# A third buffer for the split expert tiles, and end keys kept in the buffer of the inverse decays

## The chip, the core and the metric

The kernel runs on one core of a Trainium2 chip. The metric is device time in microseconds (us), the median of repeated runs. One more execution was recorded by the hardware profiler; all rows below come from it, and the times in them count from the start of its span. Engines: PE is the matrix engine (TensorE), PEld its weight loads, DVE is VectorE, ACT is ScalarE, POOL is GpSimd, SP issues DMAs.

## The reference

Three layers, one after the other. First a linear attention with decay over 4 batches, 8 heads, 768 tokens and a head width of 48:

```
for t in range(S):
    cur = einsum('bhd,bhe->bhde', u * k[t], v[t])
    y[t] = einsum('bhd,bhde->bhe', r[t], state + cur)
    state = w[t][..., None] * state + einsum('bhd,bhe->bhde', k[t], v[t])
```

Its output, 3072 tokens by 384, goes through a first expert, and that one's output through a second:

```
h = x @ w_in;  e = exp(h - max(h));  solu = h * e / (sum(e) + 1e-9)      # 384 -> 1024
x = ((solu - mean) / sqrt(var + 1e-6) * g_ln) @ w_out                    # 1024 -> 384
h = x @ w_in2; out = maximum(0.01 * h, h) @ w_out2                       # 384 -> 2048 -> 384
```

## The kernel before

**Tiles and stages.** The attention is worked in 24 chunks of 128 tokens (6 per batch), m counting them. Three chunks form a super tile of 384 tokens, which is what the experts' matmuls stream. One super tile takes 24 steps on PE: 8 steps of the kind M1 (the second matmul of the first expert) and 16 of the kind M2 (the second expert). f is the step within its kind, fp numbers all steps of a batch.

**A step.** `prod` writes a tile of 128 features by 384 tokens into one of two PSUM banks, PR[fp % 2]: in M2 nine matmuls of X2 by w_in2 (a product in high and low parts, so three matmuls for each of three blocks), in M1 three transposes of LN. ACT and DVE then split the tile into a high part RH and a low part RL:

- M2, four operations in a chain: ACT writes 0.01 times the tile to Rraw (L693), DVE takes the maximum with the tile (L967), ACT rounds that to RH (L697), DVE writes the rest to RL (L974). Rraw and RL are the same memory.
- M1, two operations: ACT writes gain times the tile to RH (L699), DVE writes the rest to RL (L976).

`cons` multiplies RH and RL by w_out (nine matmuls, summed in the banks ACC) and counts up the semaphore pe_cons. PE's order is prod(fp), cons(fp-2), prod(fp+1), cons(fp-1), and so on; at the end of the M1 steps, and after the last step of all, the pending cons are done in a row. RH, RL and Rraw have two buffers, fp % 2, so ACT's first operation on a tile has two waits (L690 and L691):

```
wait(act, pe_prod, steps(b, fp))
wait(act, pe_cons, steps(b, fp - 2))
```

**The attention beside the steps.** The work of a chunk is cut into 8 slots, which lists written in the program hang between the steps, several per step in the first 16 M2 steps (the opening). For chunk m the slots have: the masked scores A on DVE (L848, slot 4), the product with A on PE (slot 5), the sum y on DVE (L861, slot 6), its transposes on PE (L1155, slot 7), the split of x (ACT L649 and DVE XL L885, slot 7), and the first matmul of the first expert, `expert_in`, 18 matmuls of 512 columns (slot 8). Behind it PE transposes the end keys of the next chunk (L1162). The maximum of the rows (L892, L895), the exponentials on ACT (L625) and their product with h on DVE (L902) follow in slot 8; in an M2 step ACT issues its L693 before that L625.

**Decays, inverse decays, end keys.** For the next chunk DVE writes the running product of the decays (`decay`, L827), its inverse ki (`inverse`, L835, four instructions), and keys times ki into the keys (`undecayed_keys`, L840). After that ACT reads ki and the decays once each to sum them up, with `junk` as the unused output (`take_range`, L656), and POOL writes keys times the last decay into a tile of its own, ke (`end_keys`, L506), which PE transposes.

**The opening.** Weights are split into high and low parts while the first steps run. ACT writes the high parts (L621) and DVE the low parts (`low_part`, L985, two operands read from SBUF, 768 columns at a time), of which the last are written in the first 16 M2 steps.

Each engine has one queue, worked in order, and all waits are semaphores written by hand.

Of the kernel before, what the change touches and what calls it, by code (L numbers as in the profile page):

```python
# [96 lines left out]
def build(nc, rkw, r_tok, k_tok, v_tok, u, w_in1, w_out1, g_ln, w_in2, w_out2,  # L97
          r_ch, k_ch, w_ch, v_ch, u_ch, y_pair, out):
    with ExitStack() as ctx:
# [36 lines left out]
        RH = sb("RH", [128, 2, ST], F32R)  # L136
        RL = sb("RL", [128, 2, ST], F32R)
        Rraw = sb("Rraw", [128, 2, ST], F32, over="RL")
# [11 lines left out]
        ke = sb("ke", [PD, PAIRS, CH])  # L150
        ki = sb("ki", [PD, PAIRS, CH])
        junk = sb("junk", [PD, PAIRS, CH])
# [61 lines left out]
        def decays(b, m):  # L214
            return part(2, b, m)

# [278 lines left out]
        def _(pool):  # L495
# [6 lines left out]
            def end_keys(b, m):  # L502
                wait(pool, dve_keys, chunks(b, m, PAIRS, PAIRS))
                wait(pool, pe_keT, chunks(b, m))
                last = decays(b, m)[:, :, CH - 1:CH].broadcast_to([PD, PAIRS, CH])
                nc.gpsimd.tensor_tensor(ke[:, :, :], keys(b, m), last, ALU.mult).then_inc(pool_ke, 1)  # L506
# [108 lines left out]
        def _(act):  # L615
# [35 lines left out]
            def take_range(b, m):  # L651

                wait(act, dve_inv, chunks(b, m, PAIRS, PAIRS))
                for i, part in enumerate((ki[:, :, :], decays(b, m))):
                    wait(act, act_range, chunks(b, m, 2, i))
                    nc.scalar.activation(junk[:, :, :], part, ACT.Copy,  # L656
                                         accum_out=spread[:, bass.ds(chunks(b, m, 2, i), 1)]).then_inc(act_range, 1)
# [29 lines left out]
            def step(b, kind, so, f, fp, m, s):  # L687
                if kind == "M1":
                    item_mid(b, m, s)
                wait(act, pe_prod, steps(b, fp))  # L690
                wait(act, pe_cons, steps(b, fp - 2))  # L691
                if kind == "M2":
                    nc.scalar.activation(Rraw[:, fp % 2, :], PR[fp % 2][:, 0:ST], ACT.Copy,  # L693
                                         scale=0.01).then_inc(act_slope, 1)
                    item_mid(b, m, s)
                    wait(act, dve_relu, supers(b, so, F2, f + 1))
                    nc.scalar.activation(RH[:, fp % 2, :], Rraw[:, fp % 2, :], ACT.Copy).then_inc(act_hi, 1)  # L697
                else:
                    nc.scalar.activation(RH[:, fp % 2, :], PR[fp % 2][:, 0:ST], ACT.Identity,  # L699
                                         scale=gain[:, f:f + 1]).then_inc(act_hi, 1)  # L700
# [118 lines left out]
        def _(dve):  # L819
# [11 lines left out]
            def inverse(b, m, a):  # L831
                if a == 0:
                    wait(dve, act_range, chunks(b, m, 2))
                wait(dve, dve_decay, chunks(b, m, PAIRS, a + 1))
                nc.vector.reciprocal(ki[:, a, :], decays(b, m)[:, a, :]).then_inc(dve_inv, 1)  # L835
# [129 lines left out]
            def step_relu(b, so, f, fp):  # L965
                wait(dve, act_slope, supers(b, so, F2, f + 1))
                nc.vector.tensor_tensor(Rraw[:, fp % 2, :], PR[fp % 2][:, 0:ST], Rraw[:, fp % 2, :],  # L967
                                        ALU.max).then_inc(dve_relu, 1)

            def step_lo(b, kind, f, fp):  # L970
                wait(dve, act_hi, marks(b, fp))
                hi = RH[:, fp % 2, :].bitcast(F32)
                if kind == "M2":
                    nc.vector.tensor_tensor(RL[:, fp % 2, :], Rraw[:, fp % 2, :], hi, ALU.subtract).then_inc(dve_lo, 1)  # L974
                else:
                    nc.vector.scalar_tensor_tensor(RL[:, fp % 2, :], PR[fp % 2][:, 0:ST], gain[:, f:f + 1], hi,  # L976
# [159 lines left out]
        def _(pe):  # L1136
# [22 lines left out]
            def transpose_keys(b, m):  # L1159
                wait(pe, pool_ke, chunks(b, m, 1, 1))  # L1160
                for a in range(PAIRS):
                    last = nc.tensor.transpose(keys_of(b, m)[:, a * PD:(a + 1) * PD], ke[:, a, :], ident[0:PD, 0:PD])  # L1162
# [167 lines left out]
            def cons(b, kind, so, f, fp):  # L1330
# [6 lines left out]
                for m in range(KM):  # L1337
# [5 lines left out]
                    for i, (w, x) in enumerate((HH, LH, HL)):  # L1343
                        last = mm(ACC[m][:, 0:ST], weights[w][:, f, m * 128:(m + 1) * 128],
                                  (RH, RL)[x][:, fp % 2, :], f == 0 and i == 0, f == tiles - 1 and i == 2)
# [118 lines left out]
```

## Time and profile before

| what | value |
|---|---|
| median of 3 runs | 805.15 us (804.94 to 806.25) |
| the profiled execution's own time | 804.72 us |
| its span, first to last instruction | 802.7 us |
| PE busy | 782.0 us, 97% of the span |
| DVE, ACT, POOL busy | 533.8 us (66%), 344.5 us (43%), 178.3 us (22%) |
| mean granted TensorE clock | 0.996 |

The busy shares are means over the whole program. PE's matmuls are pipelined: the length shown for one (0.34 us for 384 columns) overlaps the next one's, and two starts are about 0.17 us apart. A row's bracket tells how long its engine sat idle before it, and what ended that. Because ends of matmuls are modelled, a short wait of PE shows better in the distance between two starts than in the bracket.

### The profile page before, as it was taken

What the parts mean: (1) busy time and instruction counts of PE and PEld (TensorE: products, weight loads), DVE (VectorE), ACT (ScalarE), POOL (GpSimd) and SP (SyncE); (2) the same over time, 40 slices, a digit from 0 to 9 for tenths busy, and PEclk for the clock granted to TensorE, in tenths of its full rate; (3) what the DMA queues carried; (4) which work ended last, traced back from release to release, by engine and by line L of the source; (5) the groups of instructions that cost most, each with busy time, mean ns of one, the idle gap of its engine ahead of it and who ended that gap; (6) DMA issues with size and microseconds to landing.
All of it is one profiled execution on the core that took longest, in us unless ns stands there. A gap on an engine that the chain in (4) does not pass through costs nothing.

```text
span 802.7 us, 12113 instructions
## 1 busy us (share of the span) xinstructions
PE 782.0 (97%) x4624; PEld 736.1 (92%) x4624; DVE 533.8 (66%) x1023; ACT 344.5 (43%) x676; POOL 178.3 (22%) x199
## 2 busy tenths in 40 slices
PE   5999999999999999999999999999999999999996
PEld 4769988899999999999999999999999999999996
DVE  6788989865668657667666676576675765553332
ACT  3386554444344343353443444345334444334332
POOL 4524313222213302222212122122221221100000
PEclk9999999999999999999999999999999999999999
DMA  9940222032021121030220311203202020000000
GB/s 274 324 173 5 62 65 65 1 94 65 1 65 39 56 65 35 30 94 1 65 65 1 95 31 34 65 1 94 65 1 65 16 79 30 1 0 30 1 1 33
DMA packets 19377, 45.88 MB, mean 57 GB/s; under 512 B 1920, under 2 KB 14336, under 8 KB 18928
## 3 DMA queue, kind: packets, MB, share of 16 engines
q1 hardware_dynamic: 15664, 37.17, 15.5%
q10 hardware_dynamic: 3648, 7.87, 2.9%
q8 instruction: 38, 0.62, 0.3%
q14 instruction: 27, 0.22, 0.1%
HBM read 40.31 MB, written 4.72 MB: 56 GB/s over the span
## 4 chain that ended last, share of the span: by engine, by line
PE 79%; DVE 1%; ACT 0%; issue 0%; DVEq 0%; ACTq 0%
PE BANKS L1138 55%; PE MISC L1138 20%; PE BANKS L1317 2%; PE MISC L1162 1%; PE MISC L1155 1%; DVE att L827 0%; DVE Rraw L967 0%; DVE RL L974 0%; ACT RH L697 0%; ACT Rraw L693 0%; DVE ki L835 0%; DVE X2L L991 0%; DVE A L848 0%; ACT X2H L714 0%; ACT OUT L720 0%
## 5 line engine op out<-in xcount | busy, mean ns | idle before, releaser
L693 ACT ACTIVATE Rraw<-BANKS 128x384 f32<-128x384 f32 x128 | 63.0, 492 | 217.7 <-PE BANKS L1138 217.5
L967 DVE TENSOR_TENSOR Rraw<-BANKS,Rraw 128x384 f32<-128x384 f32 x128 | 71.1, 555 | 118.8 <-ACT Rraw L693 118.7
L1138 PE MATMUL BANKS<-RH,W4H 128*128 128x384 f32 x384 | 136.1, 354 | 0.9 <-DVE RL L974 0.8
L1138 PE MATMUL BANKS<-X2H,W3H 128*128 128x384 f32 x384 | 130.7, 340 | 0.2 <-DVE X2L L991 0.2
L1138 PE MATMUL BANKS<-RH,W4L 128*128 128x384 f32 x384 | 129.8, 338 | 0.0
L1138 PE MATMUL BANKS<-RL,W4H 128*128 128x384 f32 x384 | 129.5, 337 | 0.0
L1138 PE MATMUL BANKS<-X2L,W3H 128*128 128x384 f32 x384 | 129.4, 337 | 0.0
L1138 PE MATMUL BANKS<-X2H,W3L 128*128 128x384 f32 x384 | 129.2, 336 | 0.0
L697 ACT ACTIVATE RH<-Rraw 128x384 fp32r<-128x384 f32 x128 | 67.2, 525 | 94.3 <-DVE Rraw L967 94.3
L974 DVE TENSOR_TENSOR RL<-Rraw,RH 128x384 fp32r<-128x384 f32 x128 | 79.3, 619 | 22.5 <-ACT RH L697 22.5
L835 DVE RECIPROCAL ki<-att 112x128 f32<-112x128 f32 x96 | 89.4, 938 | 0.0
L506 POOL TENSOR_TENSOR ke<-att 112x512 f32<-112x512 f32 x24 | 32.3, 1345 | 197.4 <-DVE att L840 197.4
L1138 PEld LDWEIGHTS BANKS<-RH,W4H 128*128 128x128 f32 x384 | 72.6, 189 | 1.8 <-DVE RL L974 1.5
L1138 PEld LDWEIGHTS BANKS<-RH,W4L 128*128 128x128 f32 x384 | 72.8, 189 | 0.3
L1138 PEld LDWEIGHTS BANKS<-X2H,W3H 128*128 128x128 f32 x384 | 72.1, 188 | 0.6 <-issue 0.5
L1138 PEld LDWEIGHTS BANKS<-RL,W4H 128*128 128x128 f32 x384 | 72.5, 189 | 0.0
L1138 PEld LDWEIGHTS BANKS<-X2H,W3L 128*128 128x128 f32 x384 | 72.1, 188 | 0.1
L1138 PEld LDWEIGHTS BANKS<-X2L,W3H 128*128 128x128 f32 x384 | 72.1, 188 | 0.0
L530 POOL TENSOR_TENSOR rstd<-vare,mhalf 128x1 f32<-128x1 f32 x24 | 14.8, 617 | 257.2 <-DVE vare L922 257.2
L892 DVE TENSOR_REDUCE hmax<-MISC 128x1 f32<-128x512 f32 x44 | 30.1, 690 | 50.8 <-PE MISC L1138 50.8
L1138 PE MATMUL BANKS<-RH,W2H 128*128 128x384 f32 x168 | 61.9, 368 | 0.0
L976 DVE SCALAR_TENSOR_TENSOR RL<-BANKS,gain,RH 128x384 fp32r<-128x384 f32 x56 | 34.5, 615 | 38.4 <-ACT RH L699 37.9
(132 smaller groups left out, 1490.0 us busy)
## 6 DMA issues: line engine op xcount, KB each, us to landing
att<-rkw SPq DMA_DIRECT2D x23, 672.0 KB, 5.0
out<-OUT SPq DMA_DIRECT2D x8, 576.0 KB, 6.4
rtok<-r_tok SPq DMA_DIRECT2D x22, 192.0 KB, 4.8
ktok<-k_tok SPq DMA_DIRECT2D x22, 192.0 KB, 4.6
vtok<-v_tok SPq DMA_DIRECT2D x22, 192.0 KB, 4.9
W3raw<-w_in ACTq DMA_DIRECT2D x1, 3072.0 KB, 18.0
W4raw<-w_out ACTq DMA_DIRECT2D x1, 3072.0 KB, 17.3
W1raw<-w_in SPq DMA_DIRECT2D x2, 768.0 KB, 11.2
```

Of the source, the lines that this page charges most:

```text
L506: nc.gpsimd.tensor_tensor(ke[:, :, :], keys(b, m), last, ALU.mult).then_inc(pool_ke, 1)
L530: nc.gpsimd.tensor_tensor(rstd[:, :], vare[:, :], mhalf[:, :], ALU.pow).then_inc(pool_rstd, 1)
L693: nc.scalar.activation(Rraw[:, fp % 2, :], PR[fp % 2][:, 0:ST], ACT.Copy, scale=0.01).then_inc(act_slope, 1)
L697: nc.scalar.activation(RH[:, fp % 2, :], Rraw[:, fp % 2, :], ACT.Copy).then_inc(act_hi, 1)
L835: nc.vector.reciprocal(ki[:, a, :], decays(b, m)[:, a, :]).then_inc(dve_inv, 1)
L892: nc.vector.reduce_max(hmax[:, n:n + 1], hidden(b, m)[:, n * 512:(n + 1) * 512], AX.X).then_inc(dve_max, 1)
L967: nc.vector.tensor_tensor(Rraw[:, fp % 2, :], PR[fp % 2][:, 0:ST], Rraw[:, fp % 2, :], ALU.max).then_inc(dve_relu, 1)
L974: nc.vector.tensor_tensor(RL[:, fp % 2, :], Rraw[:, fp % 2, :], hi, ALU.subtract).then_inc(dve_lo, 1)
L976: nc.vector.scalar_tensor_tensor(RL[:, fp % 2, :], PR[fp % 2][:, 0:ST], gain[:, f:f + 1], hi, ALU.mult, ALU.subtract).then_inc(dve_lo, 1)
L1138: return nc.tensor.matmul(dst, lhsT, rhs, start=start, stop=stop, skip_group_check=True)
L1155: last = nc.tensor.transpose(XT[:, k * CH:(k + 1) * CH], tokens(0, b, m)[:, k * 128:(k + 1) * 128], ident[:, :])
L1317: last = nc.tensor.transpose(dst[:, c * CH:(c + 1) * CH], LN[:, c, f * 128:(f + 1) * 128], ident[:, :])
```

## The change

RH, RL and Rraw get three buffers, fp % 3, and ACT's first operation on a tile waits for cons of fp - 3 in place of fp - 2. The tile ke goes. The end keys of chunks 0 to 2 are written into first_ke, which lies over a part of W4H not yet in use; those of chunk 3 into junk; those of all later chunks into ki. For this three waits are added. POOL's end keys wait until ACT has read ki of that chunk (for chunk 3: until ACT has written junk twice). ACT's sums of chunk 4 wait for the transposed end keys of chunk 3. DVE's first inverse of chunk 5 and later waits until PE has transposed the end keys of the chunk before. Every engine has the same instructions in the same order as before; only names and waits differ.

```diff
-        RH = sb("RH", [128, 2, ST], F32R)
-        RL = sb("RL", [128, 2, ST], F32R)
-        Rraw = sb("Rraw", [128, 2, ST], F32, over="RL")
+        RH = sb("RH", [128, 3, ST], F32R)
+        RL = sb("RL", [128, 3, ST], F32R)
+        Rraw = sb("Rraw", [128, 3, ST], F32, over="RL")
-        ke = sb("ke", [PD, PAIRS, CH])
         ki = sb("ki", [PD, PAIRS, CH])
+        later_ke = sb("ke", [PD, PAIRS, CH], over="ki")
+        first_ke = sb("first_ke", [PD, PAIRS, CH], over="W4H", skip=F2 * MODEL // 8 * 8)
         junk = sb("junk", [PD, PAIRS, CH])
...
+        def ke(b, m):
+            if first(b, m):
+                return first_ke
+            return junk if first(b, m - 1) else later_ke
...
                 wait(pool, pe_keT, chunks(b, m))
                 last = decays(b, m)[:, :, CH - 1:CH].broadcast_to([PD, PAIRS, CH])
-                nc.gpsimd.tensor_tensor(ke[:, :, :], keys(b, m), last, ALU.mult).then_inc(pool_ke, 1)
+                if not first(b, m):
+                    wait(pool, act_range, chunks(b, m, 2, 2 if first(b, m - 1) else 1))
+                nc.gpsimd.tensor_tensor(ke(b, m)[:, :, :], keys(b, m), last, ALU.mult).then_inc(pool_ke, 1)
...
                 wait(act, dve_inv, chunks(b, m, PAIRS, PAIRS))
+                if first(b, m - 2) and not first(b, m - 1):
+                    wait(act, pe_keT, chunks(b, m))
...
                 wait(act, pe_prod, steps(b, fp))
-                wait(act, pe_cons, steps(b, fp - 2))
+                wait(act, pe_cons, steps(b, fp - 3))
                 if kind == "M2":
-                    nc.scalar.activation(Rraw[:, fp % 2, :], PR[fp % 2][:, 0:ST], ACT.Copy,
+                    nc.scalar.activation(Rraw[:, fp % 3, :], PR[fp % 2][:, 0:ST], ACT.Copy,
                                          scale=0.01).then_inc(act_slope, 1)
...
             def inverse(b, m, a):
                 if a == 0:
                     wait(dve, act_range, chunks(b, m, 2))
+                if a == 0 and not first(b, m - 2):
+                    wait(dve, pe_keT, chunks(b, m))
```

The other lines of the diff turn fp % 2 into fp % 3 where RH, RL or Rraw are read or written, and ke into ke(b, m) in PE's transposes.

## Rows read from the trace of the kernel before

**Rows 1.** Three stretches: busy us (instructions) per engine, TensorE clock, DMA share, GB/s
```profile
200.00:250.00 50.00, 50.00 (x296) 48.49 (x295) 34.20 (x69) 20.65 (x40) 11.41 (x12) 1.00 0.09 27
110.00:150.00 40.00, 39.21 (x220) 36.27 (x220) 35.35 (x65) 19.48 (x37) 10.43 (x11) 1.00 0.12 37
155.00:158.50 3.50, 3.50 (x15) 3.40 (x14) 3.44 (x4) 0.29 (x1) 0.43 (x1) 0.51 0.00 0
```
**Rows 2.** PE's waits from 20 to 160 us: total us, times, longest
```profile
PE MISC L1138 <- DVE XL L885: 1.2, 2, 0.8
```
**Rows 3.** PE in order of time, the opening's end: start, length, names [idle before <-releaser]
```profile
152.39 1.96 PE L1138 MATMUL MISC<-vtok,A 128*128 128x48 f32 x16 [1.45 <-DVE A L848]
...
154.96 0.60 PE L1138 MATMUL BANKS<-RH,W4H 128*128 128x384 f32 x1
...
160.40 0.49 PE L1155 MATMUL MISC<-ident,rtok 128*128 128x128 f32 x3
```
**Rows 4.** ACT in order of time: its first operation on three tiles
```profile
89.54 0.49 ACT L693 ACTIVATE Rraw<-BANKS 128x384 f32<-128x384 f32 x1 [1.09 <-PE BANKS L1138]
...
142.53 0.49 ACT L693 ACTIVATE Rraw<-BANKS 128x384 f32<-128x384 f32 x1 [1.11 <-PE BANKS L1138]
...
158.21 0.58 ACT L699 ACTIVATE RH<-BANKS,gain 128x384 fp32r<-128x384 f32 x1 [3.89 <-PE BANKS L1138]
```
**Rows 5.** DVE in order of time: its waits for those operations, and what follows
```profile
88.98 0.21 DVE L895 TENSOR_SCALAR nmax<-hmax 128x1 f32<-128x1 f32 x1
90.06 0.56 DVE L967 TENSOR_TENSOR Rraw<-BANKS,Rraw 128x384 f32<-128x384 f32 x1 [0.86 <-ACT Rraw L693]
...
116.77 0.56 DVE L967 TENSOR_TENSOR Rraw<-BANKS,Rraw 128x384 f32<-128x384 f32 x1 [1.44 <-ACT Rraw L693]
...
143.06 0.56 DVE L967 TENSOR_TENSOR Rraw<-BANKS,Rraw 128x384 f32<-128x384 f32 x1 [1.46 <-ACT Rraw L693]
...
151.62 1.22 DVE L848 TENSOR_TENSOR A<-MISC,causal 128x512 f32<-128x512 f32 x2
...
158.83 0.62 DVE L976 SCALAR_TENSOR_TENSOR RL<-BANKS,gain,RH 128x384 fp32r<-128x384 f32 x1 [0.39 <-ACT RH L699]
159.36 0.55 DVE L861 TENSOR_TENSOR rtok<-MISC,rtok 128x384 f32<-128x384 f32 x1
```
**Rows 6.** The last super tile, ACT: first operation on an M2 stage's last tile
```profile
725.99 0.49 ACT L693 ACTIVATE Rraw<-BANKS 128x384 f32<-128x384 f32 x1 [0.40 <-PE BANKS L1138]
...
792.08 0.49 ACT L693 ACTIVATE Rraw<-BANKS 128x384 f32<-128x384 f32 x1 [1.48 <-PE BANKS L1138]
```
**Rows 7.** PE in order of time, the last two cons of the program
```profile
793.21 0.34 PE L1138 MATMUL BANKS<-RL,W4H 128*128 128x384 f32 x1
794.37 0.44 PE L1138 MATMUL BANKS<-RH,W4H 128*128 128x384 f32 x1 [0.82 <-DVE RL L974]
```
**Rows 8.** The chain of waits, 728 to 737 us: start, us, what
```profile
730.11 0.33 PE BANKS L1317 x3
730.44 1.58 PE BANKS L1138 x9
```
**Rows 9.** End keys of chunk 6: ACT, POOL, DVE and PE, in order of time
```profile
136.87 0.62 ACT L656 ACTIVATE junk<-ki 112x512 f32<-112x512 f32 x1
...
137.08 1.38 POOL L506 TENSOR_TENSOR ke<-att 112x512 f32<-112x512 f32 x1 [7.92 <-DVE att L840]
...
137.47 1.81 DVE L985 TENSOR_TENSOR W3L<-W3raw,W3H 128x768 fp32r<-128x768 f32 x1
...
140.29 0.55 PE L1162 MATMUL MISC<-ident,ke 112*128 112x112 f32 x4
```
**Rows 10.** End keys of chunk 3 (POOL), of chunk 20 (POOL, PE)
```profile
64.69 3.44 POOL L506 TENSOR_TENSOR ke<-att 112x512 f32<-112x512 f32 x1 [0.63 <-DVE att L840]
...
576.66 1.38 POOL L506 TENSOR_TENSOR ke<-att 112x512 f32<-112x512 f32 x1 [10.10 <-DVE att L840]
...
580.43 0.55 PE L1162 MATMUL MISC<-ident,ke 112*128 112x112 f32 x4
```

More of the change, by code:

```diff
@@ L696, in step @@
                     wait(act, dve_relu, supers(b, so, F2, f + 1))
-                    nc.scalar.activation(RH[:, fp % 2, :], Rraw[:, fp % 2, :], ACT.Copy).then_inc(act_hi, 1)
+                    nc.scalar.activation(RH[:, fp % 3, :], Rraw[:, fp % 3, :], ACT.Copy).then_inc(act_hi, 1)
                 else:
-                    nc.scalar.activation(RH[:, fp % 2, :], PR[fp % 2][:, 0:ST], ACT.Identity,
+                    nc.scalar.activation(RH[:, fp % 3, :], PR[fp % 2][:, 0:ST], ACT.Identity,
                                          scale=gain[:, f:f + 1]).then_inc(act_hi, 1)
@@ L966, in step_relu @@
                 wait(dve, act_slope, supers(b, so, F2, f + 1))
-                nc.vector.tensor_tensor(Rraw[:, fp % 2, :], PR[fp % 2][:, 0:ST], Rraw[:, fp % 2, :],
+                nc.vector.tensor_tensor(Rraw[:, fp % 3, :], PR[fp % 2][:, 0:ST], Rraw[:, fp % 3, :],
                                         ALU.max).then_inc(dve_relu, 1)
@@ L971, in step_lo @@
                 wait(dve, act_hi, marks(b, fp))
-                hi = RH[:, fp % 2, :].bitcast(F32)
+                hi = RH[:, fp % 3, :].bitcast(F32)
                 if kind == "M2":
-                    nc.vector.tensor_tensor(RL[:, fp % 2, :], Rraw[:, fp % 2, :], hi, ALU.subtract).then_inc(dve_lo, 1)
+                    nc.vector.tensor_tensor(RL[:, fp % 3, :], Rraw[:, fp % 3, :], hi, ALU.subtract).then_inc(dve_lo, 1)
                 else:
-                    nc.vector.scalar_tensor_tensor(RL[:, fp % 2, :], PR[fp % 2][:, 0:ST], gain[:, f:f + 1], hi,
+                    nc.vector.scalar_tensor_tensor(RL[:, fp % 3, :], PR[fp % 2][:, 0:ST], gain[:, f:f + 1], hi,
                                                    ALU.mult, ALU.subtract).then_inc(dve_lo, 1)
@@ L1161, in transpose_keys @@
                 for a in range(PAIRS):
-                    last = nc.tensor.transpose(keys_of(b, m)[:, a * PD:(a + 1) * PD], ke[:, a, :], ident[0:PD, 0:PD])
+                    last = nc.tensor.transpose(keys_of(b, m)[:, a * PD:(a + 1) * PD], ke(b, m)[:, a, :], ident[0:PD, 0:PD])
                 last.then_inc(pe_keT, 1)
@@ L1344, in cons @@
                         last = mm(ACC[m][:, 0:ST], weights[w][:, f, m * 128:(m + 1) * 128],
-                                  (RH, RL)[x][:, fp % 2, :], f == 0 and i == 0, f == tiles - 1 and i == 2)
+                                  (RH, RL)[x][:, fp % 3, :], f == 0 and i == 0, f == tiles - 1 and i == 2)
                     if f == tiles - 1 and m < KM - 1:
```

## The prediction

> **What bounds the kernel now.** I read the stretches first, then PE's waits, then the four engines side by side where PE waits, and the chain of waits near the end. In the stretch from 200 to 250 us PE is busy for all 50.00 us [rows 1]. So a buffer more can give nothing there: its matmuls are the time. The other stretches between 167 and 725 us read alike. What can be won lies where PE waits behind the two-buffer rule, and that is at two places.
>
> The first is the opening's end. From 110 to 150 us PE is busy 39.21 of 40 us while DVE is busy 35.35 [rows 1]. PE waits twice for XL, 1.2 us together [rows 2], and 1.45 us for the masked scores A [rows 3]. Both are DVE's. In this stretch DVE writes the last low parts of the weights and is nearly full, but it also idles: 0.86, 1.44 and 1.46 us before L967 [rows 5]. These waits come behind the slots with `expert_in`, and they are for ACT's first operation (L693). ACT in turn sat idle 1.09 us before it, released by PE [rows 4]; the tile had been written before `expert_in`, more than 4 us earlier, so what ACT waits for is cons of fp - 2. This is the wait that the change moves. It happens three times in the opening (steps 3, 8 and 13; of the middle one, 116.25 us with 1.09 us idle, only DVE's side is in the rows).
>
> The second place is the very end. The last tile's L693 starts at 792.08 after 1.48 us of idleness [rows 6], and PE starts the last cons 0.82 us late by the bracket, at 794.37, 1.16 us after the start before it; nine matmuls take 1.58, so 0.17 apart is their normal distance [rows 7, 8]. By starts the wait is 0.99, so a bracket tells 0.17 too little.
>
> **The opening, step by step.** With fp - 3 the cons in question was done long ago, so L693 starts when ACT is free: 1.09, 1.09 and 1.11 us earlier than now, counted against PE [rows 4].
>
> - Step 3: L693 could start at 88.45. DVE's L967 started at 90.06 and DVE was free at about 89.2, when nmax was done (88.98 and 0.21) [rows 5], so L967 gains 0.86. But DVE's next operation waits for the exponentials, which ACT issues behind L693 and which need nmax. They start some 0.4 us after L693, now at about 89.9, and with nmax done at 89.19 and a semaphore behind it at 89.3 at the earliest. That makes 0.63 us for DVE and all behind it.
> - PE's first wait for XL then goes: DVE is 0.63 earlier, and of the 1.2 us for two waits the longest was 0.8 [rows 2], so this one is 0.4, and 0.6 with the 0.17. PE is 0.6 earlier from there on.
> - Step 8: L693 comes 0.62 (PE's own gain) plus 1.09 earlier, 1.71 in all. DVE had 1.44 idle there beside the 0.63 already won [rows 5], room for 2.07, so it takes the whole 1.71.
> - PE's second wait for XL (0.8, and 0.97 with the 0.17) goes, and PE is about 1.57 earlier.
> - Step 13: L693 comes 1.57 + 1.11 = 2.68 earlier. DVE has room for 1.71 + 1.46 = 3.17, so it takes 2.68.
> - DVE is busy without a gap from there to A, so A starts at 148.94 instead of 151.62 [rows 5]. PE is ready 1.57 earlier, at about 149.4, and still waits for A: about 0.3 us in place of 1.45 by its bracket. PE's row at 152.39 [rows 3] moves to 149.7. **Gain so far: 2.68.**
>
> **The clock after it.** From 155.00 to 158.50 the granted clock was 0.51 [rows 1], that is the 1.2 GHz level; it fell 2.6 us after PE's longest wait of the stretch. From PE's start at 154.96 to the transposes at 160.40 are two cons and two sets of three transposes [rows 3]: 5.44 us, where two times 1.58 + 0.33 [rows 8] are 3.82. So the low clock cost about 1.6 us. The two shorter waits, 1.2 us together, were followed by no fall (clock 1.00 from 110 to 150) [rows 1]. If 0.3 us of waiting is left, I expect no fall. But not all of the 1.6 comes back, because DVE is next: the transposes at 160.40 need y (L861 at 159.36, 0.55 long) [rows 5]. DVE comes there 2.68 earlier, plus 0.39 that it now idles before L976, whose ACT operation waited 3.89 us for a cons [rows 4, 5] and will be early. So y is ready at 156.84 and PE's transposes start at about 156.94: 3.46 earlier than now. **The opening gives 3.46**; 2.68 if the clock falls as before. Later DVE has room again (34.20 of 50 us from 200 on [rows 1]), and PE keeps what it has.
>
> **The end.** The last L693 waits only for its own product, one cons (1.58) earlier, at about 790.5 [rows 6, 8]. PE's start at 794.37 then comes 0.17 behind 793.21: 1.16 - 0.17 = **0.99** gained [rows 7], since the chain of four moves by more than that. At the last stage change from M2 to M1 (725.99) ACT idled 0.40 [rows 6]; nothing to 0.40 can come of it, and I take 0.37, as the chain from L693 to cons has no other work in between. The other changes of stage have slots of the attention between, and PE does not wait there.
>
> **What the new waits cost.** POOL's end keys now wait for ACT's first read of ki. For chunk 6 that read runs from 136.87 to 137.49, its sum to about 137.7, while POOL started at 137.08 [rows 9]: 0.6 us later. PE's transposes follow at 140.29 and the end keys were done at 138.46, so 1.83 us of room hide it; for chunk 20 it is 576.66 + 1.38 = 578.04 against 580.43, 2.39 of room [rows 9, 10]. Nothing else of POOL is due behind it. All chunks from 4 on have this shape. Chunk 3's end keys (64.69) [rows 10] wait for both of ACT's writes of junk, which follow within some 2.3 us; they took 3.44 beside three weight operations, and PE's transposes of them lie behind the scores of chunk 3, some 3 us after 64.69 + 3.44: I take nothing, at most 0.5. ACT's new wait and DVE's ask for transposes that PE has done at least a slot and a whole step before: nothing. As instructions the added waits are bounded by 0 and some 0.1 us each on DVE; of the three in the opening I take nothing, as DVE's starts follow each other without a visible gap for the two waits that it has. Moving the buffers in SBUF costs nothing that a row shows.
>
> One thing speaks against the later end keys. DVE's W3L took 1.81 us beside them: from 137.47 it ran 0.99 us until they ended at 138.46, and then the 0.8 to 0.9 that such an operation takes [rows 9]. The Trainium skill (SBUF — State Buffer, "Who interferes with whom") has this as an exclusive lock on a port pair that DVE and GpSimd share, held for the whole instruction by whoever starts first. By that rule, the trace agrees, end keys that start 0.6 us later find DVE already holding the pair and are blocked in their turn, perhaps by two weight operations, which uses up 1.4 to 1.8 of the 1.83 us of room. The sum would be 0.1 to 0.3 us smaller by it; its greater weight is with the slower rival.
>
> **The sum.** 3.46 + 0.99 + 0.37 = 4.82. The profiled execution took 804.72, so it would take 799.9; its time lies 0.43 under the median of the runs, 805.15, and from the median the forecast is 800.3.
>
> **Rivals.**
>
> - The clock falls all the same (it need not have been the wait that brought it down). Then the opening gives 2.68: 805.15 - 4.04 = 801.1. For it: the trace has one fall only, which proves no cause. Chance 0.2.
> - DVE doesn't convert it: another wait ends just behind L693 (PE's transposed end keys into keT on ACT, or the exponentials), or DVE's weight operations and POOL's collide anew and eat the 2 to 3 us before A. Only the end is left, 1.36: 803.8. Against it: ACT's idleness of 1.09 is measured behind keT, and DVE's room was larger than the gain twice out of three. Chance 0.1.
> - The change doesn't do what it says: PR has still two banks, and if these and not cons of fp - 2 hold ACT and PE, all stays at 805.1. Against it: the 1.48 us idle before 792.08 [rows 6] is one cons long. Chance 0.04.
> - Slower: the end keys come too late for PE in every chunk. Those of chunk 3 took 3.44 us beside DVE's weight operations [rows 10]. If the 0.6 us shift puts each into such company, they end 0.6 + 3.44 - 1.38 = 2.66 us later than now. That is 0.83 too late in each of three opening chunks (room 1.83) and 0.27 in 17 others (room 2.39) [rows 9, 10]: 2.5 + 4.6 = 7.1 us lost, 805.15 - 4.82 + 7.1 = 807.4. It decides once end keys end more than 2.4 us later than now; 2 us later costs only half a microsecond in the opening. Against it: outside the opening DVE is busy 34.20 of 50 us [rows 1], and its single operations are mostly under 1 us. Chance 0.06.
>
> **The numbers.** The forecast has 0.6. Its own range is 799.3 to 801.0. With the clock rival and part of the third the range for 8 in 10 is 799.0 to 802.6. A measurement of this kernel can tell about 0.2%, 1.6 us, from no change, so faster means below 803.5: forecast and clock rival, and a few hundredths of the rest, 0.82. Within 0.2%: 0.11 (the third and fourth rival mostly). Slower by more than 0.2%: 0.07.
>
> **What would show it.** In the profile after, PE should have no wait for XL, at most 0.5 us for A, at about 149.7, and the clock 1.00 from 155 to 158; DVE's idleness before L967 in the opening should be gone or under 0.5 us; ACT should wait for PE before its first operation only until the product is there; the last cons should follow without a bracket. The end keys should start 0.6 us after where they did against DVE's keys, and PE should never wait for them. A PE wait on L1162, or a new one between 85 and 165 us that isn't named here, would prove the sum wrong; PE busy below 50.00 in a stretch after 200 us would prove the reading of the rest wrong.

## The result, and the profile after

| | before | after |
|---|---|---|
| median of the runs, us | 805.1 (804.94 to 806.25) | 796.18 (795.36 to 796.56, 4 runs) |
| the profiled execution, us | 804.72 | 795.36 |
| its span, us | 802.7 | 793.3 |
| ratio, after to before | | 0.9882, 95% interval [0.9869, 0.9895] |

The change makes the kernel 9.5 us faster by the ratio (interval 8.5 to 10.5), 8.9 us by the two medians. I forecast 800.3 with a range from 799.0 to 802.6: the direction was right and the gain about half of what came.

Line numbers moved: PE's L1138 is now L1150, L1317 is L1329, L1162 is L1174; ACT's L693, L697 and L699 are L703, L707 and L709; DVE's L967, L974, L976 are L979, L986, L988. The stretches first (busy us and instructions of each engine, clock, DMA):

```profile
110.00:150.00 40.00, 39.63 (x227) 37.12 (x225) 37.50 (x68) 19.58 (x38) 12.47 (x12) 1.00 0.12 35
155.00:158.50 3.50, 3.24 (x21) 2.77 (x20) 3.50 (x7) 2.90 (x7) 0.00 (x0) 1.00 0.11 18
200.00:250.00 50.00, 50.00 (x307) 48.64 (x306) 34.34 (x72) 19.47 (x37) 13.19 (x14) 1.00 0.09 27
```

Beside [rows 1], PE gained 0.42 us of work between 110 and 150 us and DVE 2.15. The clock is 1.00 after 155. The third row holds 50.00 busy microseconds as before, but 307 instructions where [rows 1] has 296: those are partly other instructions, since everything moved by 4 us, but a share of busy time that stands at 100% in both can't tell whether something was won there. PE's rows at the two waits that it has around the opening's end:

```profile
149.96 1.96 PE L1150 MATMUL MISC<-vtok,A 128*128 128x48 f32 x16 [0.36 <-DVE A L860]
...
156.50 0.55 PE L1329 MATMUL BANKS<-ident,LN 128*128 128x128 f32 x3 [0.26 <-DVE RL L988]
```

The two waits for XL [rows 2] are gone, and that for A fell from 1.45 to 0.36 [rows 3]. The small one for RL of the next stage isn't in the first profile of the kernel before. But the change did not bring it: the second profile of that kernel (experiment 8), whose clock did not fall here, has it too:

```profile
159.41 0.55 PE L1317 MATMUL BANKS<-ident,LN 128*128 128x128 f32 x3 [0.23 <-DVE RL L976]
```

DVE in the opening:

```profile
85.38 0.95 DVE L997 TENSOR_TENSOR W4L<-W4raw,W4H 128x768 fp32r<-128x768 f32 x1
86.25 1.81 DVE L997 TENSOR_TENSOR W3L<-W3raw,W3H 128x768 fp32r<-128x768 f32 x1
...
89.81 0.56 DVE L979 TENSOR_TENSOR Rraw<-BANKS,Rraw 128x384 f32<-128x384 f32 x1 [0.30 <-ACT Rraw L703]
...
115.59 0.56 DVE L979 TENSOR_TENSOR Rraw<-BANKS,Rraw 128x384 f32<-128x384 f32 x1 [0.40 <-ACT Rraw L703]
...
140.63 0.56 DVE L979 TENSOR_TENSOR Rraw<-BANKS,Rraw 128x384 f32<-128x384 f32 x1 [0.23 <-ACT Rraw L703]
...
149.19 1.22 DVE L860 TENSOR_TENSOR A<-MISC,causal 128x512 f32<-128x512 f32 x2
```

Its idleness of 0.86, 1.44 and 1.46 us [rows 5] is 0.30, 0.40 and 0.23. The very end on PE, where [rows 7] shows a bracket of 0.82:

```profile
784.95 0.34 PE L1150 MATMUL BANKS<-RL,W4H 128*128 128x384 f32 x1
785.13 0.33 PE L1150 MATMUL BANKS<-RH,W4H 128*128 128x384 f32 x1
```

But for the wait for RL all this is as forecast. What was not forecast is in the chain of waits at a change of stage from M2 to M1, in the middle of the kernel where I had promised nothing. Before (start, us, what):

```profile
446.39 1.57 PE BANKS L1138 x9
...
448.62 2.04 PE BANKS L1138 x9
```

After:

```profile
440.92 1.57 PE BANKS L1150 x9
...
443.14 1.57 PE BANKS L1150 x9
```

The first cons of the M1 stage, nine matmuls as any other, took 2.04 us in the chain before and takes 1.57 now. PE has no idle bracket there in either trace. The starts tell it. PE before:

```profile
448.13 0.49 PE L1155 MATMUL MISC<-ident,rtok 128*128 128x128 f32 x3
448.58 0.41 PE L1138 MATMUL BANKS<-RH,W2H 128*128 128x384 f32 x1
...
449.52 0.34 PE L1138 MATMUL BANKS<-RL,W2H 128*128 128x384 f32 x1
449.86 0.44 PE L1138 MATMUL BANKS<-RH,W2H 128*128 128x384 f32 x1
```

and after:

```profile
442.65 0.49 PE L1167 MATMUL MISC<-ident,rtok 128*128 128x128 f32 x3
442.90 0.42 PE L1150 MATMUL BANKS<-RH,W2H 128*128 128x384 f32 x1
...
444.03 0.34 PE L1150 MATMUL BANKS<-RH,W2H 128*128 128x384 f32 x1
```

From the transposes to the cons it is 0.45 us before and 0.25 after, and the third group of three follows after 0.34 us instead of the 0.17 that is normal. A matmul's recorded length (0.34) is twice the distance at which the next can start (0.17). So a wait of up to some 0.17 us leaves no idle time in the record, and several of them in a row add up unseen. What PE waited for stands on ACT. Before:

```profile
446.17 0.58 ACT L699 ACTIVATE RH<-BANKS,gain 128x384 fp32r<-128x384 f32 x1 [3.54 <-PE BANKS L1138]
446.65 1.27 ACT L642 ACTIVATE rb<-att 48x512 f32<-48x512 f32 x2
447.94 0.87 ACT L720 ACTIVATE OUT<-BANKS 128x384 f32<-128x384 f32 x2
448.84 0.58 ACT L699 ACTIVATE RH<-BANKS,gain 128x384 fp32r<-128x384 f32 x1
449.32 0.48 ACT L720 ACTIVATE OUT<-BANKS 128x384 f32<-128x384 f32 x1
```

After:

```profile
435.60 0.58 ACT L709 ACTIVATE RH<-BANKS,gain 128x384 fp32r<-128x384 f32 x1 [0.25 <-PE BANKS L1329]
436.08 1.27 ACT L650 ACTIVATE rb<-att 48x512 f32<-48x512 f32 x2
441.54 0.95 ACT L730 ACTIVATE OUT<-BANKS 128x384 f32<-128x384 f32 x2 [4.19 <-PE BANKS L1150]
```

The M1 stage's cons overwrites the banks from which ACT copies OUT. Before, ACT stood 3.54 us at RH of the first M1 tile, waiting for cons of fp - 2. RH, two rotations of keys and only then the copies of OUT came behind it, and PE asked for these bank by bank. With three buffers RH and the rotations are done by 437.35 us, and ACT has idled 4.19 us when the accumulators are complete (441.54). That PE's hidden waits are for the copies of OUT is an inference from these rows. Experiment 6, which moves the copies alone, bears it out.

To put a price on it I compare the start of the same matmul in two traces: each has 4624, in one order. Distances below are counted from a matmul at about 32 us, so that the noise of the first loads stays out. The kernel to compare with is the first experiment, which has all of the change but the distance.

| place | forecast | changed kernel against the first experiment |
|---|---|---|
| up to A (150 us) | 2.68 | 3.36 |
| clock and y behind it | 0.78 | 0 |
| first cons of M1, five changes of stage (257, 352, 448, 543, 640 us) | 0 | 0.55 to 0.62 each, 2.9 in all |
| thirteen other places, 0.09 each | 0 | 1.2 |
| the sixth change (726 us) | 0.37 | 0.36 |
| the last cons | 0.99 | 1.12 |
| a faster pace from 750 to 790 us, at no single start | 0 | 0.77 (the kernel before has it too) |
| the rest, in steps of at most 0.02 each | 0 | 0.2 |

The thirteen places are always the same two: the first transposes of LN for an M1 stage, some 8 us ahead of its first cons (six times), and the second matmul of the last cons of an M1 stage (seven times). Here are PE's rows at the latter, before:

```profile
276.57 0.43 PE L1138 MATMUL BANKS<-RH,W2H 128*128 128x384 f32 x1
276.84 0.34 PE L1138 MATMUL BANKS<-RH,W2L 128*128 128x384 f32 x1
```

and in experiment 4, which has the distance of three here:

```profile
273.32 0.34 PE L1150 MATMUL BANKS<-RH,W2H 128*128 128x384 f32 x1
273.50 0.33 PE L1150 MATMUL BANKS<-RH,W2L 128*128 128x384 f32 x1
```

The distance is 0.27 us before and 0.18 there. All thirteen are gone in the five traces with the distance of three in all M2 tiles and in the M1 tiles behind the first (the changed kernel, experiments 4, 5, 10 and 11). They are there in the other eight (one measures 0.03 us in four of these traces, and two 0.06 in experiment 9). So they belong to the moved wait. What PE waits for at them isn't shown.

The pace is another matter. From 750 to 790 us PE does nothing but matmuls of 384 columns at a clock of 1.00, and yet it starts 233 of them in the first profile of the kernel before and 229 in the second:

```profile
750.00:790.00 40.00, 40.00 (x233) 40.00 (x232) 14.48 (x26) 12.74 (x26) 0.00 (x0) 1.00 0.01 1
750.00:790.00 40.00, 40.00 (x229) 40.00 (x228) 13.85 (x25) 12.71 (x25) 0.00 (x0) 1.00 0.01 1
```

The same 231 distances take 40.04 us in three traces (the kernel before, the changed one, experiment 11) and 40.81 us in the other ten. The kernel before has both paces in its two profiles, so the change isn't needed for the faster one. Whether it makes it likelier, so few profiles can't tell.

### The profile page after: what moved, and what is told of

It reads as the page before. It is cut to its first block, busy times and chain, and to the rows that moved or that the text cites. A ratio compares the mean times of both kernels' runs of the same rounds, so it can differ in the third digit from the quotient of the medians.

```text
span 793.3 us, 12113 instructions
## 1 busy us (share of the span) xinstructions
PE 775.5 (98%) x4624; PEld 735.6 (93%) x4624; DVE 520.8 (66%) x1023; ACT 341.3 (43%) x676; POOL 173.2 (22%) x199
## 4 chain that ended last, share of the span: by engine, by line
PE 79%; DVE 1%; issue 0%; ACT 0%; DVEq 0%
PE BANKS L1150 55%; PE MISC L1150 20%; PE BANKS L1329 2%; PE MISC L1174 1%; PE MISC L1167 1%; DVE ki L847 0%; DVE W2L L997 0%; DVE att L837 0%; DVE A L860 0%; DVE Rraw L979 0%; DVE RL L986 0%; DVE X2L L1003 0%; ACT X2H L724 0%; ACT OUT L730 0%; DVE diag L867 0%
## 5 line engine op out<-in xcount | busy, mean ns | idle before, releaser
L1150 PE MATMUL BANKS<-RH,W4H 128*128 128x384 f32 x384 | 135.5, 353 | 0.0
L1150 PE MATMUL BANKS<-X2H,W3H 128*128 128x384 f32 x384 | 130.6, 340 | 0.2 <-DVE X2L L1003 0.2
L1150 PE MATMUL BANKS<-X2L,W3H 128*128 128x384 f32 x384 | 129.4, 337 | 0.0
L1150 PE MATMUL BANKS<-X2H,W3L 128*128 128x384 f32 x384 | 129.2, 336 | 0.0
L1150 PE MATMUL BANKS<-RH,W4L 128*128 128x384 f32 x384 | 129.1, 336 | 0.0
L1150 PE MATMUL BANKS<-RL,W4H 128*128 128x384 f32 x384 | 129.0, 336 | 0.0
L979 DVE TENSOR_TENSOR Rraw<-BANKS,Rraw 128x384 f32<-128x384 f32 x128 | 70.8, 553 | 87.4 <-ACT Rraw L703 86.5
L703 ACT ACTIVATE Rraw<-BANKS 128x384 f32<-128x384 f32 x128 | 62.6, 489 | 137.4 <-PE BANKS L1150 137.1
L707 ACT ACTIVATE RH<-Rraw 128x384 fp32r<-128x384 f32 x128 | 67.1, 524 | 101.5 <-DVE Rraw L979 101.5
L986 DVE TENSOR_TENSOR RL<-Rraw,RH 128x384 fp32r<-128x384 f32 x128 | 71.1, 556 | 22.5 <-ACT RH L707 22.5
L1150 PEld LDWEIGHTS BANKS<-X2H,W3H 128*128 128x128 f32 x384 | 72.1, 188 | 0.6 <-issue 0.5
L1150 PEld LDWEIGHTS BANKS<-RH,W4L 128*128 128x128 f32 x384 | 72.4, 188 | 0.3
L1150 PEld LDWEIGHTS BANKS<-RH,W4H 128*128 128x128 f32 x384 | 72.2, 188 | 0.3
L1150 PEld LDWEIGHTS BANKS<-X2H,W3L 128*128 128x128 f32 x384 | 72.1, 188 | 0.1
L1150 PEld LDWEIGHTS BANKS<-X2L,W3H 128*128 128x128 f32 x384 | 72.1, 188 | 0.0
L1150 PEld LDWEIGHTS BANKS<-RL,W4H 128*128 128x128 f32 x384 | 72.1, 188 | 0.0
L514 POOL TENSOR_TENSOR ke<-att 112x512 f32<-112x512 f32 x20 | 22.7, 1133 | 217.8 <-ACT junk L666 163.7
L1150 PE MATMUL BANKS<-RH,W2H 128*128 128x384 f32 x168 | 60.6, 361 | 0.0
L988 DVE SCALAR_TENSOR_TENSOR RL<-BANKS,gain,RH 128x384 fp32r<-128x384 f32 x56 | 33.1, 591 | 41.3 <-ACT RH L709 41.3
```

The lines of the kernel that those rows point to most:

```text
L514: nc.gpsimd.tensor_tensor(ke(b, m)[:, :, :], keys(b, m), last, ALU.mult).then_inc(pool_ke, 1)
L703: nc.scalar.activation(Rraw[:, fp % 3, :], PR[fp % 2][:, 0:ST], ACT.Copy, scale=0.01).then_inc(act_slope, 1)
L707: nc.scalar.activation(RH[:, fp % 3, :], Rraw[:, fp % 3, :], ACT.Copy).then_inc(act_hi, 1)
L979: nc.vector.tensor_tensor(Rraw[:, fp % 3, :], PR[fp % 2][:, 0:ST], Rraw[:, fp % 3, :], ALU.max).then_inc(dve_relu, 1)
L986: nc.vector.tensor_tensor(RL[:, fp % 3, :], Rraw[:, fp % 3, :], hi, ALU.subtract).then_inc(dve_lo, 1)
L988: nc.vector.scalar_tensor_tensor(RL[:, fp % 3, :], PR[fp % 2][:, 0:ST], gain[:, f:f + 1], hi, ALU.mult, ALU.subtract).then_inc(dve_lo, 1)
```

## The experiments

**1. The end keys' new places alone.** The changed kernel, with the distance put back:

```diff
-                wait(act, pe_cons, steps(b, fp - 3))
+                wait(act, pe_cons, steps(b, fp - 2))
```

> The changed kernel, but ACT's first operation on a tile waits for cons of fp - 2 as before. So the third buffer is there and never used; the end keys lie where the change puts them, with their three new waits. Theory: all of the gain comes from the moved wait, so 805 us (804.5 to 805.6), no difference from before; the end keys start 0.6 us after DVE's keys plus what they wait for ACT, and PE never waits for them. The hidden part to look at: DVE's W4L beside the end keys is 0.95 us instead of 1.81, nmax at step 3 is done about 0.6 us earlier, and DVE then waits that much longer for L703. Rival: moving the end keys is itself worth something, since they no longer block DVE in the opening: 803 to 804 us.

Measured: 804.41 us (803.57 to 805.5), before 804.88; ratio 0.9996 [0.9987, 1.0005], no difference. All of the gain that can be told from noise is the moved wait's, and the new waits, which I took at nothing, cost nothing. PE stood 1.45 us for A again, and yet:

```profile
155.00:158.50 3.50, 3.50 (x28) 3.46 (x28) 3.50 (x4) 0.94 (x3) 1.56 (x2) 1.00 0.02 5
```

The clock did not fall. The next row shows what the later end keys did by themselves: DVE waits 1.50 us for L703, where [rows 5] has 0.86. Its weight operations had gone through sooner, and the time became idleness.

```profile
91.22 0.56 DVE L979 TENSOR_TENSOR Rraw<-BANKS,Rraw 128x384 f32<-128x384 f32 x1 [1.50 <-ACT Rraw L703]
```

**2. The distance of three in the opening's M2 steps alone.**

```diff
-                wait(act, pe_cons, steps(b, fp - 3))
+                wait(act, pe_cons, steps(b, fp - (3 if opening(b, kind, so) else 2)))
```

> The changed kernel, but the wait is for cons of fp - 3 only in the 16 M2 steps of the opening, and for cons of fp - 2 everywhere else. Theory (the gain has three places: opening some 4.5 us, the five stage changes from M2 to M1 between 250 and 650 us some 0.8 each, the end 1.4): 801 us (800.3 to 801.5), no low clock after 150 us, and the stage changes as before (a cons of 2.04 us in the chain of waits). Rival (what was predicted: nothing between 167 and 725 us, so that the opening gave all that the end did not): 797.5 us.

Measured: 801.26 us (800.65 to 802.44); ratio 0.9955 [0.9943, 0.9968], 3.6 us. PE's start for A is 3.36 us earlier, as in the changed kernel, and by the starts the five changes of stage gain nothing (0.00); the long cons are still there, 2.01 to 2.03 us in the chain. The time lies in the expected range, but the opening's term, 4.5 us, was too large: it had the fall of the clock in it.

**3. The distance of three at the first tile of an M1 stage alone.**

```diff
-                wait(act, pe_cons, steps(b, fp - 3))
+                wait(act, pe_cons, steps(b, fp - (3 if kind == "M1" and f == 0 else 2)))
```

> The changed kernel, but the wait is for cons of fp - 3 only in the first M1 step of each stage (f = 0), and for cons of fp - 2 everywhere else. Theory (ACT's L699 of that step, which waited for a cons, held up the copies of ACC to OUT, and PE's next cons waited for those): the cons of 2.04 us becomes 1.57 and its neighbours shrink at each of the stage changes, 0.7 to 0.8 us each in five of them and up to 0.5 at the first: 805.1 - 4 = 801 us (800.5 to 801.8). The waits for XL and A in the opening stay. Rival: the stage changes gained by something else (all buffers, the chain of the last M2 tile): 805 us.

Measured: 802.2 us (800.94 to 806.28); ratio 0.9970 [0.9960, 0.9981], 2.4 us. By the starts each of the five changes gave 0.57, 2.84 in all, and the chain has

```profile
447.90 1.56 PE BANKS L1150 x9
```

I had expected 0.7 to 0.8 each and 801 us (at most 801.8), so the place was right and the size too large. One tile of the twenty-four in a super tile needs the third buffer here, and there lies most of what my forecast lacked.

**4. The distance of three everywhere but at that tile.**

```diff
-                wait(act, pe_cons, steps(b, fp - 3))
+                wait(act, pe_cons, steps(b, fp - (2 if kind == "M1" and f == 0 else 3)))
```

> The changed kernel, but in the first M1 step of each stage (f = 0) the wait is for cons of fp - 2. Theory: the counterpart of the run before; it loses the some 0.8 us of each middle stage change and keeps opening and end: 796.2 + 4 = 800 us (799.3 to 800.8). Rival (the last M2 tiles' earlier chain is what counts at the stage change): 796.2 us, as the changed kernel.

Measured: 798.28 us (797.17 to 799.6); ratio 0.9914 [0.9901, 0.9927]. I had expected 800 (from 799.3). The part missing to the changed kernel, 0.0032 or 2.6 us, is within the intervals what experiment 3 won alone. In the chain:

```profile
445.04 2.03 PE BANKS L1150 x9
```

The profiled execution of this kernel had a fall of the clock of its own, at another place:

```profile
42.00:50.00 8.00, 6.84 (x16) 3.86 (x17) 3.39 (x10) 7.31 (x15) 0.74 (x2) 0.57 0.89 314
...
42.20:43.20 1.00, 0.04 (x1) 0.04 (x1) 0.00 (x0) 1.00 (x2) 0.00 (x0) 0.50 1.06 372
```

By the starts this execution lost 4.2 us between 40 and 50 us, but not all of it to the clock. PE waited 3.0 us for LN from 40.1 us on, where it waits 1.7 in the other twelve, because ACT came late to its work for LN: it had waited 3.71 us for W3raw from the DMA. That is 1.3 us, and the clock fell only within this wait, at 42.2. The other 2.9 were lost while it was low. The distances from 168 us on agree with the other traces.

**5. The changed kernel with the end keys early.** ACT's sums of the range stand ahead of RH in the M2 steps, so that the end keys start as early as before and meet DVE's weight operations in the old order.

```diff
+                    if early_range(b, kind, m, s):
+                        take_range(b, m + 1)
                     item_mid(b, m, s)
                     wait(act, dve_relu, supers(b, so, F2, f + 1))
...
-                    item_end(b, m, s, attend)
+                    item_end(b, m, s, attend, early_range(b, kind, m, s))
```

> The changed kernel, but in M2 steps ACT reads ki and the decays for its sums (L656 before, L666 after) ahead of the step's RH instead of behind it, so that POOL's end keys need not wait for ACT and start right behind DVE's keys, as in the kernel before. Theory (the opening gained 0.7 us more than forecast because the delayed end keys let DVE's weight operation go first): W4L beside the end keys takes 1.81 us again, nmax of step 3 is done about 0.6 us later against the steps, and PE's product with A comes 0.5 to 0.8 us later than in the changed kernel; 796.9 us (796.2 to 797.6). Rival (the surplus comes from the moved wait alone): PE's start of the product with A stays where it is in the changed kernel, 796.2 us, though W4L is 1.81 us.

Measured: 796.38 us (795.88 to 796.7); ratio 0.9886 [0.9863, 0.9908], the changed kernel's own. W4L is long again, and ACT's exponentials now wait for nmax:

```profile
85.72 1.81 DVE L1002 TENSOR_TENSOR W4L<-W4raw,W4H 128x768 fp32r<-128x768 f32 x1
...
90.53 1.12 ACT L633 ACTIVATE EXP<-MISC,nmax 128x1024 f32<-128x1024 f32 x1 [0.38 <-DVE nmax L912]
```

Counted on DVE, step 3 gives 0.68 us here (the forecast had 0.63) and 1.20 with the late end keys; step 8 gives 1.31 and 0.93; A comes 3.23 us earlier here and 3.38 there. So of the half a microsecond that the late end keys win at step 3 most is lost again at step 8. A comes 0.15 us later here, where the theory had 0.5 to 0.8: the surplus of the opening is the moved wait's, as the rival had it, but for those 0.15 us.

**6. Two buffers, the copies of OUT ahead of the items.** In the second M1 step of a stage:

```diff
-                    if out_due and f == 2:
-                        take_out(b, so - 1, (KM - 1,))
+                    if out_due and f == 1:
+                        take_out(b, so - 1)
                     for at, t in items:
                         item(b, at, t)
-                    if out_due and f == 1:
-                        take_out(b, so - 1, range(KM - 1))
```

> The kernel of e1 (two buffers' wait, fp - 2, everywhere) with one move: in the second M1 step of a stage (f = 1) ACT issues all three copies of ACC to OUT (L720 before) ahead of the step's other work, instead of two behind it and one in the next step. If PE's hidden waits at the stage changes are for these copies, which are late because ACT's L699 waits for a cons and stands ahead of them, they go without a third buffer: the cons of 2.04 us in the chain of waits becomes 1.57, 0.5 to 0.7 us at each of the seven changes, 804.6 - 4 = 800.6 us (800 to 802). Rival (PE waits for RL of the first M1 tile itself, which fp - 3 brings earlier): the cons stays 2.04 us, 804.4 us.

Measured: 807.49 us (806.72 to 809.33); ratio 1.0027 [1.0016, 1.0039]. Neither time that I had given came. The first cons of an M1 stage lost its 0.45 us over 1.57 and went down to about 1.57 us, as the mechanism wants: what PE waited for there are the copies of OUT. But this step's RH now stood behind the copies and the rotations, and PE waited for its RL:

```profile
451.17 0.58 ACT L709 ACTIVATE RH<-BANKS,gain 128x384 fp32r<-128x384 f32 x1
```

```profile
452.45 0.55 PE L1327 MATMUL BANKS<-ident,LN 128*128 128x128 f32 x3 [0.79 <-DVE RL L986]
```

There is such a wait at each of the five changes of stage, and with it a change costs 0.6 us more than it did.

**7. The distance of three at the program's last tile alone.**

```diff
-                wait(act, pe_cons, steps(b, fp - 3))
+                last_tile = isinstance(b, int) and b == B - 1 and fp == SPB_STEPS
+                wait(act, pe_cons, steps(b, fp - (3 if last_tile else 2)))
```

> The changed kernel with the wait for cons of fp - 3 only at the very last M2 tile, and fp - 2 everywhere else. Theory: PE's 0.82 us bracket before the last cons goes, 0.99 us by starts: 803.6 us (803.2 to 804.2) where e1 had 804.4. Rival (an earlier L703 alone changes nothing, PE waits for another): 804.4 us.

Measured: 803.43 us (802.02 to 805.16); ratio 0.9976 [0.9964, 0.9989]. By the starts the last cons gained 1.02 us, as expected.

**8. The kernel before, once more.**

> The kernel before once more, for its profile. If the low clock after 155 us belongs to PE's wait of 1.45 us for A, it is there again. If not, as e1 and e3 had that wait and no low clock, it comes in some executions only: then some 1.2 us of the difference between the two first profiles is no effect of the change.

Measured: 804.78 us, and PE waited 1.46 us for A as it did the first time. Behind it:

```profile
155.00:158.50 3.50, 3.50 (x26) 3.46 (x25) 3.50 (x5) 1.12 (x3) 0.90 (x1) 1.00 0.00 0
```

The fall in the first profile is not a consequence of that wait alone. By the starts it cost 1.25 us net there. The repeat saved them and still took as long, because later starts fell back by 0.87 us: 0.77 of it is the slower pace between 750 and 790 us.

**9. Two buffers, the copies of OUT, then RH, then the items.**

```diff
+                    behind = out_due and f == 1
+                    if behind:
+                        take_out(b, so - 1)
                     for at, t in items:
+                        if not behind:
+                            item(b, at, t)
                     step(b, kind, so, f, fp, m, s)
+                    for at, t in items:
+                        if behind:
+                            item(b, at, t)
...
```

> The end keys as in the changed kernel, the wait for cons of fp - 2 kept (two tiles' distance everywhere), and in the second M1 step of a stage ACT's order is written anew: the three copies of OUT, then this step's RH, then the sums of the range and the rotated keys. Theory (each stage change lost 0.6 us because RH of the first M1 tile waited for a cons and the copies of OUT came behind it and two rotations of the keys): the first cons of an M1 stage falls from 2.04 to about 1.57 us in the chain and no other wait comes for it, so five stage changes give 0.57 each, 2.8 us: about 802.0 against 804.8. Rival (ACT's work at the stage change needs its time wherever it stands, and only a third buffer frees it, since what ACT does not wait for at the first tile it waits for at the second): PE waits for RL or for the keys in the second step instead, as it did with the copies first alone, and the time is 804.4 or more.

Measured: 807.43 us (806.38 to 808.51); ratio 1.0037 [1.0022, 1.0052]. The rival was right. RL is in time now at the changes of stage, and the rotations are what is late: XH and XL behind them hold PE in the next step, five times again. The chain of waits and PE's row:

```profile
448.76 0.58 ACT RH L709
449.34 0.51 ACT rb L650
...
450.53 0.50 ACT XH L657
...
451.06 0.57 DVE XL L900
```

```profile
451.67 0.50 PE L1153 MATMUL MISC<-W1H,XH 128*128 128x512 f32 x1 [0.78 <-DVE XL L900]
```

**10. The changed kernel, two low parts of W2 later.** They move from the opening's slot 15 into the third and fourth step of the M1 stage behind it.

```diff
-              11: ((3, 6), (1, 1)), 12: ((2, 7), (3, 7)), 15: ((1, 2), (1, 3))}
+              11: ((3, 6), (1, 1)), 12: ((2, 7), (3, 7)), }
...
+                    if isinstance(b, int) and b == 0 and kind == "M1" and so == 1 and f in (2, 3):
+                        low_part(1, f)
```

> The changed kernel, with two of DVE's low parts of W2 (groups 2 and 3, about 0.8 us each or more) moved from the opening's slot 15 into the third and fourth step of the first M1 stage. Theory (after the change the opening's end is bound by DVE: PE still waits 0.36 us by the bracket for A and 0.3 for RL): the wait for RL of the first M1 tile at about 156 us goes (0.42 by starts), the wait for A stays, since the two operations stand behind it; about 795.8 against 796.2. Rival (ACT's RH or the mask's own length sets this wait): unchanged at 796.2. Slower rival: the moved parts, now beside PE's rows of the first M1 stage, make RL of the fourth tile late by up to one operation: 796.6 to 797.

Measured: 795.76 us (795.19 to 796.32); ratio 0.9887 [0.9872, 0.9902], no difference from the changed kernel. At 157 us PE is 0.6 us ahead of the changed kernel, and by 173 us all but 0.14 of it is gone. The chain shows where it went:

```profile
167.65 0.87 DVE W2L L997
168.51 0.54 DVE RL L988
...
169.09 0.55 PE BANKS L1331 x3
```

A moved low part now stands ahead of an RL for which PE waits. The theory held for the wait at 156 us. What the slower rival described came too, but it cost only what had been won: 795.76 us is not its 796.6 to 797, and it can't be told from the theory's 795.8 or from no change.

**11. The changed kernel, once more.**

> The changed kernel once more, for a second profile. Theory (the slow clock after 155 us in the first profile of the kernel before was chance, and the chain of PE's starts repeats from execution to execution): PE's start for A lies again 3.2 to 3.5 us and the start of the last M1 stage 9 us ahead of the kernel before, counted from the same matmul at 32 us, except for a fall of the clock at some other place, and a total of about 796 us. Rival (falls of the clock are set by what the kernel does): a fall at the same place as in another profile of this kernel, or none, in every one.

Measured: 794.61 us. A comes 3.36 us earlier (3.38 in the first profile), and the five changes of stage give the same. The clock is 1.00 until PE's work ends. The two profiles of this kernel show no fall of the clock, and of the kernel before one does and one doesn't. So the same program can do either. Between the changes of stage the pace differs a little, and by 722 us this execution is 0.71 us ahead of the other of the same kernel. A sum of starts over the whole length can be off by as much. A jump at one matmul can be read far more closely: experiments 1, 2 and 8, whose waits are the same from 168 to 790 us, keep their distance there to 0.06 us.

## Why the prediction was wrong

**The reading of the middle failed.** The step was: "In the stretch from 200 to 250 us PE is busy for all 50.00 us [rows 1]. So a buffer more can give nothing there: its matmuls are the time." The busy time of PE is made of modelled ends that overlap the next start, so 50.00 of 50 allows waits. Five changes of stage held nearly 0.6 us each: 2.84 us in experiment 3 by itself, 2.9 in the changed kernel. Thirteen other places held 0.09 us each, 1.2 in all, and stretches of 50.00 of 50 hid these as well. The same step misread the changes of stage a second time: "PE does not wait there". I took the sixth from ACT's bracket at L693 [rows 6], an M2 tile, and looked at no L699 of an M1 tile, although [rows 4] has one with 3.89 us of idleness in front. Nor could my sign of a wrong reading, PE busy below 50.00 in a stretch after 200 us, have shown it. The view that would have told is the one that I used for the normal price of a cons [rows 8]: the same nine matmuls stand there with 2.03 or 2.04 us at 448.62 and at each of the four other changes.

**The opening was mis-sized by 0.7 us: 3.38 measured against 2.68.** The mechanism and its three places were right. Step 3 alone would have been 0.63 as I worked out (0.68 in experiment 5). What was too small is PE's own gain, from which steps 8 and 13 follow: 0.93 us by 116 us and 2.14 by 142, where I had 0.6 and 1.57. The two waits for XL gave 0.62 and 0.95 by the starts, as foreseen (0.57 and 0.97). The rest, 0.57 us by 142 us, I had not in the sum: 0.20 us at the first matmuls of the scores in each of two chunks, and 0.11 and 0.06 at the matmul behind each wait for XL. These are again waits that no bracket shows.

**The clock and the limit by y: 0.78 forecast, nothing found.** That the low clock is absent after the change is right, and it was absent from a repeat of the kernel before too, with the same wait for A. So it isn't a gain of the change. In the two first profiles the difference is in the times (starts 4.62 us apart at 168 us instead of 3.38), in the medians it is not. Here I let one execution's accident into the sum. What limits PE next is not y, as I had it, but RL of the M1 tile (0.26 us by its bracket). The kernel before waits for it too where its clock stays up (0.23 us in experiment 8).

**The end was right:** 0.99 forecast; 1.12 in the changed kernel, 1.02 in experiment 7. So was the sixth change: 0.37 forecast, 0.36 measured.

**The new waits cost nothing, as said.** Experiment 1 is within 0.2% of before. The end keys start 0.66 us later against DVE's keys, 0.6 forecast. Of the slower rival, that they would be blocked in their turn, a fifth of a microsecond came: 1.59 us where [rows 9] has 1.38.

```profile
85.65 1.59 POOL L514 TENSOR_TENSOR ke<-att 112x512 f32<-112x512 f32 x1 [9.42 <-ACT junk L666]
```

They end at 87.24, and PE's transposes of them start at 88.27. The Trainium skill (SBUF — State Buffer, "Who interferes with whom") has DVE and GpSimd lock a shared port pair against each other. The trace agrees on both sides. Whichever weight operation meets the end keys takes 1.81 us, and the one free of them 0.95. The end keys take 1.05 us where no weight operation runs (at 159.81 in the changed kernel); at 85.65 they meet W4L, which has 0.6 us to go, and take 1.59. By that length they were held up by one operation and not by two. I had written that by the rule the sum would be 0.1 to 0.3 us smaller. Experiment 1 shows no such loss, and in experiment 5 the early end keys bring A not earlier but 0.15 us later.

**The sum by measured terms:** 3.36 + 2.9 + 1.2 + 0.36 + 1.12 = 8.9 us, against 4.82 forecast and 9.5 measured (8.5 to 10.5); the two medians differ by 8.9. So nothing clear of noise is left over. Three parts by themselves, experiments 2, 3 and 7, won 0.45, 0.30 and 0.24%, together 0.99% or 8.0 us, each give or take 0.1%; by the starts they are 3.36 + 2.84 + 1.02 = 7.2, and neither the thirteen places nor the sixth change is among them. The distances of starts differ by 9.9 us between the changed kernel and experiment 1. The last 1.0 of these comes in steps of at most 0.02 us, and the kernel before has 0.77 of it as well.

Experiments 6 and 9 show why the order alone doesn't do it. With two buffers, RH of the first M1 tile starts when cons of fp - 2 is done, and 0.85 us later the first bank of OUT is complete (447.65 and 448.50 us in experiment 6). RH takes 0.48 of them, and the two rotations would take another 1.27: they don't fit. Put behind the copies they delay RL or XL, put ahead they delay OUT. With three buffers RH and the rotations are done before the last cons begins.

## What to carry to other kernels

Where PE reads 100% busy, compare the price of equal pieces in the chain of waits, or the distances between starts. A group of nine that takes 2.04 us at one place and 1.57 elsewhere is a wait, whatever the busy share says.

A wait that sits far from the bottleneck is worth what is queued behind it on its engine. To price a looser wait, go through each kind of tile that passes that line and ask what stands behind it, not only those where the bracket touches the critical engine.

A feature of one execution (a dip of the clock, a pace) isn't a term of a sum until a second one shows it.

## What the runs showed of the hardware

While PE had work, the granted clock fell in two of the thirteen profiles, at two places: to 0.51 over 3.5 us from 155 us on, that is the 1.2 GHz level, and to a mean of 0.57 from 42 to 50 us. The first came 2.6 us after PE had waited 1.45 us; the same wait (1.4 to 1.5 us) in experiments 1, 3, 6, 7, 8 and 9 was followed by none. The second came within a wait of 3.0 us for LN, which is 1.7 in the other twelve. The low clock cost 1.25 us of starts the first time and 2.9 the second. What brings it down in one execution and not in the next, the traces don't tell.

Matmuls of 384 columns in a row, at a granted clock of 1.00, have one of two paces from 750 to 790 us: 231 distances take 40.04 us in three traces and 40.81 in ten, a mean of 0.173 or 0.177 us. The same kernel shows both, and the traces don't tell why.

A DVE weight operation of 128x768 takes 0.9 to 0.95 us alone and 1.81 beside POOL's end keys. Those take 1.05 us alone, 1.38 or 1.59 beside one weight operation, and 3.44 for chunk 3 before, where three weight operations followed each other [rows 10]; with their start moved behind these, they take 1.24.
